# Chunked delta-rule attention in front of two dense layers: heads paired by feature half, products over four alternating 64x64 tiles, and the order of a chunk rearranged

## The reference, cut to what matters

```python
k_n = k / (norm(k) + 1e-6)
for t in range(S):
    y[:, :, t] = einsum('bhd,bhde->bhe', q[:, :, t], state)
    v_old = einsum('bhde,bhd->bhe', state, k_n[:, :, t])
    state += beta[t] * einsum('bhd,bhe->bhde', k_n[:, :, t], v[:, :, t] - v_old)
```

## Time and profile before

| | |
|---|---|
| median of 3 runs | 892.65 us (891.03 to 893.04) |
| the profiled execution's own time | 890.82 us |
| its span, first to last instruction | 889.0 us |
| PE busy | 825.5 us (93% of the span) |
| DVE busy | 518.8 us (58%) |
| ACT busy | 343.1 us (39%) |
| POOL busy | 161.4 us (18%) |
| granted TensorE clock, mean share of full speed | 0.974 |

### The profile page before, as it was taken

How to read it: one execution, slowest core, us unless ns; L and a number is a source line. 1 busy time by engine, 2 the same in 40 slices (tenths; PEclk the granted TensorE clock), 3 DMA queues, 4 the chain that set the end, 5 groups by cost and what they waited for, 6 DMA issues and landing times.

```text
span 889.0 us, 24900 instructions
## 1 busy us (share of the span) xinstructions
PE 825.5 (93%) x11040; PEld 589.7 (66%) x11040; DVE 518.8 (58%) x1212; ACT 343.1 (39%) x659; POOL 161.4 (18%) x183
## 2 busy tenths in 40 slices
PE   5479897999989798999999999999999999999998
PEld 5479797989989555665566556665656666666664
DVE  5677768686756377362347244625554776867522
ACT  4356565556564225131314030503233453434311
POOL 5132313132210010120012001001221433323200
PEclk8699999899999899999999999999999999999999
DMA  8223423332211204101000101000000000000001
GB/s 196 54 51 69 134 49 71 70 74 58 58 39 35 78 28 138 49 1 54 1 27 27 54 1 37 18 1 1 1 1 1 1 28 10 27 18 27 28 27 54
DMA packets 60984, 37.69 MB, mean 42 GB/s; under 512 B 45641, under 2 KB 57292, under 8 KB 60876
## 3 DMA queue, kind: packets, MB, share of 16 engines
q1 hardware_dynamic: 52612, 30.95, 12.8%
q10 hardware_dynamic: 8264, 5.15, 2.2%
HBM read 26.65 MB, written 4.72 MB: 35 GB/s over the span
## 4 chain that ended last, share of the span: by engine, by line
PE 80%; DVE 7%; ACT 6%; issue 4%; DMA 1%; ACTq 1%; SPq 0%; DVEq 0%
PE bank L291 13%; PE bank L1036 5%; PE bank L1084 5%; PE bank L1082 5%; PE bank L1083 5%; PE bank L1038 5%; PE bank L1037 5%; PE bank L330 4%; PE bank L1020 3%; PE bank L1022 3%; PE bank L1021 3%; PE bank L970 2%; DVE hT_lo L1454 2%; PE bank L358 2%; PE bank L976 2%
## 5 line engine op out<-in xcount | busy, mean ns | idle before, releaser
L1202 ACT ACTIVATE hT_hi<-bank 128x384 f16<-128x384 f32 x96 | 46.8, 489 | 160.9 <-PE bank L1022 160.8
L1036 PE MATMUL bank<-wA,hT_hi 128*128 128x384 f16 x288 | 94.0, 326 | 2.8 <-DVE hT_lo L1454 2.8
L1454 DVE SCALAR_TENSOR_TENSOR hT_lo<-bank,hT_hi 128x384 f16<-128x384 f32 x96 | 53.2, 555 | 73.7 <-ACT hT_hi L1202 73.4
L1020 PE MATMUL bank<-unT,wA 128*128 128x384 f16 x288 | 93.9, 326 | 0.3 <-DVE hT_lo L1454 0.3
L1022 PE MATMUL bank<-unT,wA 128*128 128x384 f16 x288 | 93.9, 326 | 0.0
L1021 PE MATMUL bank<-unT,wA 128*128 128x384 f16 x288 | 93.9, 326 | 0.0
L1038 PE MATMUL bank<-wA,hT_lo 128*128 128x384 f16 x288 | 93.9, 326 | 0.0
L1037 PE MATMUL bank<-wA,hT_hi 128*128 128x384 f16 x288 | 93.9, 326 | 0.0
L291 PE MATMUL bank<-Yv,ET 64*64 64x48 f32 x2304 | 76.2, 220 | 6.0 <-issue 3.9
L291 PEld LDWEIGHTS bank<-Yv,ET 64*64 64x64 f32 x2304 | 71.8, 136 | 9.3 <-issue 5.2
L278 POOL TENSOR_TENSOR AP<-AP,mP 128x256 f32<-128x256 f32 x48 | 36.2, 773 | 178.4 <-ACT AP L438 178.2
(11 more groups left out here) (202 smaller groups left out, 1781.7 us busy)
## 6 DMA issues: line engine op xcount, KB each, us to landing
Kb<-k_dram SPq DMA_DIRECT2D x12, 384.0 KB, 5.5
Vv<-v_dram SPq DMA_DIRECT2D x12, 384.0 KB, 3.7
z_first<-w_dram SPq DMA_DIRECT2D x8, 576.0 KB, 4.0
z_first<-wt_dram SPq DMA_DIRECT2D x8, 576.0 KB, 3.6
out_dram<-hT_hi SPq DMA_DIRECT2D x24, 192.0 KB, 1.8
KQ<-q_dram SPq DMA_DIRECT2D x44, 96.0 KB, 4.1
X<-Yo ACTq DMA_DIRECT2D x12, 192.0 KB
X<-Yo ACTq DMA_DIRECT2D x10, 189.0 KB
```

What stands on the lines that cost most here:

```text
L1020: pe.matmul(out, w1[0][:, k, cols], unT[0][:, k, :], start=(k == 0), stop=False)
L1036: pe.matmul(out, hT[0][:, f, cols], w2[0][:, f, :], start=(f == 0), stop=False)
L1454: dve.scalar_tensor_tensor(hT[1][:, f, :], bank[3 + m % 3][:, 0:TG * P], 0.0, hT[0][:, f, :], ALU.max, ALU.subtract).then_inc(s_hl, 1)
```

## The change

A head's feature half r is now the upper or lower eight of its sixteen places (r = g // 8) instead of g % 2. The tensors KQ, Kb and the banks are laid out to suit. Products over the four tiles now go round them, (0, 0), (1, 1), (0, 1), (1, 0), with different halves r writing to different banks, and the passes and their semaphores are gone. K is loaded in rows of 1536 bytes instead of 192, Q in rows of 2048 instead of 256. The keys are turned by 32 products with a 64x64 identity instead of eight 128x128 transposes. In PE's turn, `corner(c, 0)` is put ahead of `predicted(c)`, and the state's growth comes between the two halves of the output. On DVE `mask_e(c, 0)` is ahead of `make_x`, and `norm` and `scale` move from the middle of the elimination to behind `scaled_u`. SP waits for hop 1 before loading Q and for hop 3 before loading K. The last chunk no longer grows the state.

```diff
-        KQ = sb("KQ", [P, RT, 2, HG, 2, C])
+        KQ = sb("KQ", [P, RT, 2, 2, HG, C])
-        Kb = sb("Kb", [P, RK, NG, C])
+        Kb = sb("Kb", [P, RK, 2, KW])          # KW = HG * D + BLK
-        STRAIGHT, CROSSED = ((0, 0), (1, 1)), ((1, 0), (0, 1))
+        TILES = ((0, 0), (1, 1), (0, 1), (1, 0))
@@ SP
                 load_v(c + 2 if c + 2 > 1 else -1)
+                if c >= 0:
+                    sp.wait_ge(s_Y, 8 * c + 4)
                 load_q(c + 3 if c + 3 > 2 else -1)
+                if c >= 0:
+                    sp.wait_ge(s_Y, 8 * c + 8)
                 load_k(c + 5 if c + 5 > 3 else -1)
@@ PE, turn
-                        mm = pe.transpose(out[:, j * P:(j + 1) * P], Kb[:, n % RK, g:g + 2].rearrange(...), ident[:])
+                for m in range(HG):
+                    for h, r in TILES:
+                        mm = pe.matmul(out[h][half[r], m * C:(m + 1) * C], key(n, h, r, m, C), ident[half[h], half[h]], ...)
@@ PE, predicted
-                for tiles in (STRAIGHT, CROSSED):
-                    for a in range(2):
...
+                pe.wait_ge(s_se, 2 * c)
+                for m in range(HG):
+                    for h, r in TILES:
+                        mm = pe.matmul(chain(r)[half[h], m * D:(m + 1) * D], KQ[feat[r], c % RT, 0, h, m],
+                                       Sv[feat[r], c % 2, h * HG + m], ...)
+                mm.then_inc(s_X, 1)
@@ PE, the order of a turn
+                corner(c, 0)
                 predicted(c)
-                corner(c, 0)
                 corner(c, 1)
                 solve(c)
-                gram(c + 2, (0, 1))
+                gram(c + 2, (0, 2))
                 hop(c, 1)
-                gram(c + 2, (2, 3))
+                gram(c + 2, (1, 3))
                 hop(c, 2)
                 turn(c + 3)
                 hop(c, 3)
-                outputs(c)
+                out = queried(c)
+                direct(c, 0, out)
+                grow(c)
+                direct(c, 1, out)
@@ ACT
             def grown(c):
+                act.wait_ge(s_S, c + 1)
                 for a in range(2):
-                    act.wait_ge(s_S, 2 * c + a + 1)
@@ DVE
+                mask_e(c, 0)
                 make_x(c)
-                mask_e(c, 0)
                 mask_e(c, 1)
                 blocks_in(c + 1)
                 eliminate(c + 1, (1, 2, 3, 4, 5, 6, 7))
                 if c < 0 and c % 2 == 0:
                     scale((c + 2) // 2)
+                eliminate(c + 1, (8, 9, 10, 11, 12, 13, 14))
+                scaled_u(c + 1)
                 if c % 2:
                     norm((c + 3) // 2)
                 elif c >= 0:
                     scale((c + 2) // 2)
-                eliminate(c + 1, (8, 9, 10, 11, 12, 13, 14))
-                scaled_u(c + 1)
                 blocks_out(c + 1)
```

More of the change, by code:

```diff
@@ L90, in attention @@
         RK, RT, RA = 6, 4, 3
+        KW = HG * D + BLK
         half = (slice(0, C), slice(C, P))
@@ L306, in turn @@
                     pe.wait_ge(s_id, 16)
[L307 to L313, removed]
+                out = [take("T", n, h) for h in range(2)]
+                for m in range(HG):
+                    for h, r in TILES:
+                        mm = pe.matmul(out[h][half[r], m * C:(m + 1) * C], key(n, h, r, m, C), ident[half[h], half[h]],
+                                       start=True, stop=True, skip_group_check=True)
+                mm.then_inc(s_T, 1)
             def gram(n, parts):
@@ L319, in gram @@
                 pe.wait_ge(s_qd[n % RT], 64 * (n // RT + 1))
-                for tiles in (STRAIGHT, CROSSED):
[L321 to L332, removed]
+                out = [take("GP", n, u) for u in parts]
+                for j in range(HG // 2):
+                    m = parts[0] * HG // 2 + j
+                    for h, r in TILES:
+                        mm = pe.matmul(out[r][half[h], j * P:(j + 1) * P], KQ[feat[r], n % RT, 0, h, m],
+                                       KQ[feat[r], n % RT, :, h, m], start=True, stop=True, skip_group_check=True)
+                mm.then_inc(s_gp, 1)
             def corner(n, u):
@@ L349, in predicted @@
                 pe.wait_ge(s_yd, 4 * c)
-                for tiles in (STRAIGHT, CROSSED):
-                    for a in range(2):
[L352 to L361, removed]
+                pe.wait_ge(s_se, 2 * c)
+                for m in range(HG):
+                    for h, r in TILES:
+                        mm = pe.matmul(chain(r)[half[h], m * D:(m + 1) * D], KQ[feat[r], c % RT, 0, h, m],
+                                       Sv[feat[r], c % 2, h * HG + m], start=m == 0, stop=True, skip_group_check=True)
+                mm.then_inc(s_X, 1)
             def solve(c):
@@ L384, in hop, with queried, direct, grow @@
                     mm.then_inc(s_Y, 1)
-            def outputs(c):
+            def queried(c):
                 if c < 0:
+                    return None
+                out = [take("O", c, a)[:, 0:HG * D].rearrange("p (g d) -> p g d", g=HG) for a in range(2)]
+                if c:
+                    for m in range(HG):
+                        for h, r in TILES:
+                            mm = pe.matmul(out[r][half[h], m], KQ[feat[r], c % RT, 1, h, m], Sv[feat[r], c % 2, h * HG + m],
+                                           start=m == 0, stop=False, skip_group_check=True)
+                    mm.then_inc(s_oq, 1)
+                return out
+            def direct(c, a, out):
+                if c < 0:
+                    return
+                pe.wait_ge(s_pt, 4 * c + 4)
+                pe.wait_ge((s_ya, s_yd)[a], 4 * c + 4)
+                if c:
+                    pe.wait_ge(s_oq, c)
+                for j in range(HG):
+                    g = a * HG + j
+                    mm = pair(out[a][:, j], PT[:, c % RA, g], Yv[:, c % 2, g], c == 0 and j == 0, True)
+                mm.then_inc(s_O, 1)
+            def grow(c):
+                if not 0 <= c < LAST:
                     return
@@ L411, in outputs @@
[L411 to L420 removed]
+                for a in range(2):
+                    pe.wait_ge((s_ya, s_yd)[a], 4 * c + 4)
@@ L422, in _ @@
+                for m in range(HG):
+                    for h, r in TILES:
+                        mm = pe.matmul(state(h)[feat[r], m * D:(m + 1) * D], key(c, h, r, m), Yv[half[h], c % 2, r * HG + m],
+                                       start=c == 0 and m == 0, stop=True, skip_group_check=True)
+                mm.then_inc(s_S, 1)
             for c in range(C0, NC):
+                corner(c, 0)
                 predicted(c)
-                corner(c, 0)
                 corner(c, 1)
                 solve(c)
-                gram(c + 2, (0, 1))
+                gram(c + 2, (0, 2))
```

78 lines of the change are left out of this document (24 added, 54 removed).

## The result

The changed kernel takes 922.69 us (median of 4 runs, 921.55 to 923.79), the kernel before 892.85 (891.03 to 894.81): ratio 1.033, 95% interval 1.031 to 1.036. It is slower by 30 us. The forecast was slower by 5.6 (898.2 us, range 883 to 908), so the direction was right and the time outside the range. The profiled execution spans 922.0 us, 33.0 more than before.

A forecast was written before the change was run, and what follows sets the result against it. Before the change, the DVE loop was taken to bound even chunks and PE mostly odd ones. Chunks 0 to 10 +7.2, chunk 11 +0.4 and start -2.0 made +5.6 us on 892.65: 898.2 us, range 883 to 908.

The forecast's parts named there:

- rival 1: In the chunks PE's clock holds at 2.4 GHz, D is 3.7 us and the kernel faster, 878 us; chance 0.17.
- Rival 2: PE bounds each odd chunk and the DVE loop is shorter than read; 871 us, chance 0.05.
- rival 3: The tiles don't run four wide, `predicted` stays at 1.85 us (3.4 at half clock); about 910 us, chance 0.08.
- D: Stretch from the corner's first product to DVE's first step of the next inverse: from 2.7 to 5.4 us.
- Chunk 11: Last chunk: -2.3 us from no growth and a hidden queries' product, +2.7 from D, together +0.4.
- The range's own terms: Upper end: D up to 6.0 (+6), scale's collisions with POOL up to 1.2 x 4, start as little as 0.
- So a chunk takes D + 11.25 + 7.05: Chunk time in DVE's loop: D 5.4, inverse 11.25, tail to next corner 7.05; 23.7 us, odd or even.
- the later growth matters in chunk 9 alone: Late growth delays Ux only in chunks without norm or scale; chunk 9, the only full one, taken as 23.0 us.
- PE's slack of 5 us a chunk: In each chunk PE, with 16.6 us of work (18 to 19 partly at half clock), stands about 5 us.
- Turning becomes 64 records for eight, 0.9 to 1.3 us: no gain, no loss.: PE's turning of the keys by small products in each chunk was priced at no change in time.
- -2.0: Ahead of the chunks: earlier small table about 1.2 us, shorter gram 0.8; -2.0 us, between -3.5 and 0.
- which the change doesn't touch: The dense part, 589.5 us, was taken as unaffected by the change.

The follow-up runs named there:

- e1: The changed kernel without SP's two new waits, so Q and K load early in a turn again: 921.4 us.
- e3: The changed kernel with `predicted` ahead of both corners on PE and `make_x` ahead of both masks on DVE, as before: 904.0 us.
- e10: The changed kernel with only the state's growth put back ahead of the output's products: 916.4 us.
- e6: e3 with the state's growth also put back ahead of the output's products: 895.2 us.
- e9: The changed kernel with only the turning altered, to 16 products of 128x64 with a 128x128 identity: 914.4 us.
- e7: e6 with keys turned by 16 products of 128x64 and ACT copying each bank once full: 885.8 us (883.1 without the disturbed run).
- e11: The kernel before with 128 already met waits on PE's queue ahead of each corner from chunk 1 on: 961.0 us.

## Why the prediction was wrong in size, step by step

The prediction's sum, made against the profiled execution, was +5.6; the profiled executions differ by +33.0. The 27.3 us between them lie in the chunks (19.6), the start (4.4), the dense part (3.1) and chunk 11 (0.2).

**What held.** The tiles run four wide: 30 records of gram took 1.07 us, 62 of the growth 0.92. The clock is half at every corner from chunk 1 on, or falls within 1.1 us of its start: rival 1 (878), which had it hold, is refuted by the granted clock of 0.87. Rival 2 (871), which needed TT in time, is refuted by PE's waits of 2.2 to 6.2 us ahead of these corners, and rival 3 by the durations above. `predicted` took 1.95 us for 62 records at half clock, where I had 1.7. D, taken as 5.4, is 5.3 to 6.0 in chunks 1 to 8, 5.7 on the mean (+2.3 in all). The norm does hold ACT's root (and by it Sv in chunks 1 and 3), and scale holds To in chunks 0 and 4. Chunk 11: +0.6 for a forecast of +0.4. The spread loads cost nothing that can be told (e1). The range's own terms (+6, +4.8 and +2.0 on 898.2) would have reached 911 and not 908 if they all came together; the measured time is above either. That the main loss comes from `predicted` between the corners is borne out by e3: 18.7 us of 30.

**The step that failed: "So a chunk takes D + 11.25 + 7.05"**, with the sentence that the later growth matters in chunk 9 alone. Chunks 1 to 8 took 205.3 us instead of 189.6:

- *The inverse was no constant.* From D to Us's end it took 11.2 to 12.2 us, 11.8 on the mean (+4.5 in all). The 11.25 had been read in chunk 10, where POOL masks nothing. Where POOL's masking of P starts just ahead of DVE's L620, as in chunks 1, 3, 4 and 8, that step and the next take 0.9 us more together; L620 took 0.99 us in chunk 3 and 0.42 in chunk 6, with nothing of POOL's beside it. The longer D isn't the reason: e3 has 12.1 to 12.2 us in chunks 1 to 7 with a D of 4.0 to 4.3, and in the kernel before the second of the two steps already took 0.84 instead of 0.43 in six chunks. The lines of chunk 3:

```profile
124.46 0.99 DVE L620 TENSOR_TENSOR Ti<-Rb,cT 128x256 f32<-128x256 f32 x1
...
124.44 1.60 POOL L285 TENSOR_TENSOR AP<-AP,mP 128x256 f32<-128x256 f32 x2 [14.47 <-ACT AP L436]
```

- *The tail, from Us's end to the next corner, was 8.2 us on the mean, not 7.05* (+8.8 in all). The growth, put behind the queries' product and half the output, ends so late that in chunks 2 and 5 to 8 Sv, and not norm or scale, sets when To can start: Sv starts 21.2 us after the corner in chunk 6, 21.5 in chunk 7 and 23.9 in chunk 2, which alone is 5.1 of the 8.8. I had priced the growth by its own duration, with PE's slack of 5 us a chunk as cover. That slack was used up ahead of it by half clock and stops. e10 puts 6.3 us on this edit, e6 8.7.
- *Scale collided* in chunk 4, as the upper end of the range had it, as POOL's squares had waited 5.87 us for K (DVE, POOL):

```profile
160.42 1.42 DVE L590 TENSOR_SCALAR cT<-cx,rows 128x32 f32<-128x32 f32 x1
161.87 1.41 DVE L591 SCALAR_TENSOR_TENSOR cT<-cx,rows,cT 128x32 f32<-128x32 f32 x1
...
160.33 1.47 POOL L264 TENSOR_TENSOR kk<-Kb 128x768 f32<-128x768 f32 x1 [5.87 <-DMA Kb<-k_dram]
```

Two steps were blocked, 2.3 us (1.42 + 1.41 - 2 x 0.25), in one of the four chunks for which I had feared it. The rest of the 19.6: chunk 0 +1.35, chunk 9 +1.55, chunk 10 +1.1.

**"Turning becomes 64 records for eight, 0.9 to 1.3 us: no gain, no loss."** Right for busy time, and wrong by 8 to 12 us against 16 larger products (e9, e7); against the eight transposes of before no run has it. I priced PE's products by their duration and never their number.

**The start, "-2.0".** It was +2.4. That the small table waits behind the short rows, and that long rows would bring it earlier, was argued, not read from a row. And gram by four tiles writes two banks a call, so that its second half waits for ACT's copies (the 0.81 us above).

**The dense part, "which the change doesn't touch".** Its first products after the handover, in the changed kernel and before:

```profile
337.38 4.19 PE L966 MATMUL bank<-fourier_tables,fourier_temps 128*128 128x385 f32 x6 [7.27 <-DVE fourier_temps L1340]
...
341.49 1.65 PE L969 MATMUL bank<-nyq,fourier_temps 1*128 1x385 f32 x2
```

```profile
306.64 4.18 PE L970 MATMUL bank<-fourier_tables,fourier_temps 128*128 128x385 f32 x6 [6.34 <-DVE fourier_temps L1344]
...
310.75 0.91 PE L973 MATMUL bank<-nyq,fourier_temps 1*128 1x385 f32 x2
```

PE waits 7.27 us for the last output's way to DVE instead of 6.34, which I put down to both halves of the last output coming together at the end now (no run tests it). Around this wait the clock is half for 13.7 us instead of 6.8 by the trace's record of the clock, 8.8 of it instead of 4.1 behind PE's first product. The two records on one partition took 1.65 us, before 0.91.

**The sum by edits**, as far as the runs give it. Undone one after another: corner order 18.7, growth 8.7, turning 9.4 us (12.1 by e7's 883.1), 36.9 in all. The change had lost 30, which is why e7 beats the kernel before. By itself each gives 18.7, 6.3 and 8.3. Norm and scale give 6.0 by themselves, just clear of the intervals, and, with the corner's order undone, -4 to -5, where the intervals overlap. What e7 gains over before was not split: beside the layout and the four tiles it has norm and scale behind the inverse, the long rows, the spread loads, turning by 16 products and no growth in the last chunk.

## What to carry to other kernels

On a chain that goes through several engines, price an edit by when its result is due, with the clock that the engine will have there, and not by its duration against an average slack. Work that is put behind other work on a queue delays everything queued after its consumer, here Sv, Ux and TT. And count instructions as well as busy time: where products of 15 to 30 ns follow each other without a pause, fewer and larger ones can win though they keep the engine busier.

## What was not expected of the hardware

- PE stops for 0.5 to 3.7 us inside a group without any wait, always at the same place in a block of 256 of its instructions, and resumes 1.2 to 1.6 us after a 16 KB instruction packet has ended. No two such packets start less than 3.2 us apart in the chunks.
- Records in four tiles can follow each other within 15 ns (62 in 0.92 us). The Trainium skill (TensorE: Matmul & The Clock Gate, Back-to-back issue gap) has a floor of about 25 ns; this trace does not show it.
- A wait that is already met costs PE's queue some 51 ns, 106 ns for an instruction with two (e11).
- DVE's small steps can wait for POOL's large ones: those of scale on 128x32, one of which took 0.25 us before, took 1.42 and 1.41 us beside POOL's squares and its scaling of V.
